# Attention tiles on TensorE: the transposes of tile n put in front of the score products of tile n+2

## The chip, the cores and the metric

The kernel runs on one core of a Trainium2 chip. The metric is the time of one execution in device microseconds (us); lower is better. The profile is one execution taken by the hardware profiler, and its times are in us from the first instruction of that execution.

## What is computed

A bucketed attention over 16 heads (2 batches of 8) with 768 positions and a head width of 64, and two dense layers behind it. Cut to what matters here:

```python
q_bits = (einsum(q, proj) > 0); k_bits = (einsum(k, proj) > 0)   # 6 bits: the bucket
mask   = q_bucket[:, None] == k_bucket[None, :]
scores = where(mask, q @ k.T / 8, -1e9)
attn   = exp(scores - max(scores)) / (sum + 1e-9)
x      = attn @ v                                                # 16 heads
x      = spatial gated MLP(x);  out = x + channel MLP(layernorm(x))
```

Products are made in three parts from high and low halves of the operands (names with h and l), so that they keep more digits than one pass would.

## The kernel before

**Tiles.** A head has 768 queries, that is T = 6 tiles of 128; the 16 heads give 96 tiles, numbered here from 0 to 95. Two heads are a pair of TILES = 12 tiles. HC = 3 tiles make half a head. Everything of the attention is written as one software pipeline over tiles, and every engine has its own fixed order of instructions, a function `steps` that goes through the tiles; engines meet only at semaphores.

**What happens to a tile n.** TensorE makes its scores (`scores`, lines L495 and L496, four matmuls of 384 columns into two banks of PSUM; tiles n and n+2 share these banks). VectorE reads them once for the negated row maximum (`maximum`, L950). ScalarE makes the exponentials into `Pe` in SBUF (`exps`, L789, signalled by `exp_done`). TensorE transposes `Pe` in six pieces (`transposes`, L526) into two banks, PT_BANK and PT_BANK+1, three pieces to a bank. ScalarE copies each bank to `PTh` (L784), rounded; VectorE subtracts to get the rest, `PTl` (`pt_lo`, L971), one instruction a bank, each of which counts `pt_split` up and so sets the bank free for the next tile's transposes. TensorE multiplies both with V (`times_v`, L538 and L540, four matmuls in most steps, for the half head before).

**The order of each engine in step n.**

- TensorE: scores of tile n+2, transposes of tile n, in some steps hash products (L505, steps with n % 6 of 1 and 2) or the turn of an output (L549, n % 3 = 0), then `times_v`.
- VectorE: maximum of tile n+2, in some steps the denominator (L977, n % 3 = 2) and the sum of the bucket bits (L963, n % 6 = 3), then `pt_lo` of tile n, and behind it the inverse (L982) and the one-hot codes of the next head (L933 at n % 6 = 1, L941 at n % 6 = 2).
- ScalarE: exponentials of tile n+1, in some steps a copy of an output (L795), `PTh` of tile n, in some steps the scaling of an output (L803).
- GpSimd splits q, k, v and the weights of the later layers; the sync engine's queue loads them.

The waits at the heart of it are these:

```python
# TensorE, transposes of tile g (n = its number in the pair)
pe.wait_ge(exp_done, g + 1)
for j in range(2):
    pe.wait_ge(pt_split, START + 2 * g + j - 1)   # VectorE is done with bank j of tile g-1
# VectorE, steps
maximum(g0 + n + 2, (n + 2) % TILES)              # waits for scores_ready of tile n+2
...
pt_lo(g0 + n, n)                                  # waits for pt_hi (PTh) of tile n
```

Before step 0 TensorE makes the scores of tiles 0 and 1; the last two steps (94 and 95) make no scores.

Of the kernel before, what the change touches and what calls it, by code (L numbers as in the profile page):

```python
# [24 lines left out]
def bucket_attention_mlp_kernel(nc, bucket_rows, qkT, qqT, kkT, v, proj, w_in, w_spT, b_sp, w_out, g_ln, w_ch, consts, out):  # L25
# [20 lines left out]
    with ctx:  # L46
        def sem(name):
            return ctx.enter_context(nc.semaphore(name))
# [152 lines left out]
        exp_done = sem("exp_done")  # L201
# [277 lines left out]
        def _(pe):  # L479
# [6 lines left out]
            def scores(n, hh):  # L486

                s, t = n // T, n % T
                if t == 0:
                    pe.wait_ge(head_split, 7 * hh + 5)  # L490
                    pe.wait_ge(coded, 2 * (hh + 1))
                tok = slice(t * P, (t + 1) * P)
                for c in range(2):
                    dst = bank[:, 2 * (n % 2) + c, 0:C]
                    nc.tensor.matmul(dst, Qs[s][:, tok], KH[s][:, c * C:(c + 1) * C], start=True, stop=False)  # L495
                    last = nc.tensor.matmul(dst, Q2[s][:, tok], KL[s][:, c * C:(c + 1) * C], start=False, stop=True)  # L496
                last.then_inc(scores_ready, 1)

            def hash_planes(hh, tiles):


                if tiles[0] == 0:
                    pe.wait_ge(qk_in, 16 * (hh + 1))
                for t in tiles:
                    last = nc.tensor.matmul(bank[:, MISC, 2 * t * NB:2 * (t + 1) * NB],  # L505
                                            qk_raw[:, bass.ds(t, P, step=T)], planes[:, :], start=True, stop=True)
                if tiles[-1] == T - 1:
                    last.then_inc(hash_mm, 1)

            def spread_buckets(hh, s):  # L510

                pe.wait_ge(buckets, hh + 1)
                for a, to in ((1, misc16), (0, o16)):
                    for t in range(T):
                        last = nc.tensor.transpose(to[:, t * P:(t + 1) * P],
                                                   cols[:, s, a, t:t + 1].to_broadcast([P, P]), ident16[:, :])
                    last.then_inc(kb_mm, 1)

            def transposes(g, n):

                pe.wait_ge(exp_done, g + 1)
                for j in range(2):
                    pe.wait_ge(pt_split, START + 2 * g + j - 1)
                    for r in range(HC):
                        k = HC * j + r
                        last = nc.tensor.transpose(bank[:, PT_BANK + j, r * P:(r + 1) * P],  # L526
                                                   Pe[n % 2][:, k * P:(k + 1) * P], ident)
                    last.then_inc(pt_ready, 1)

            def times_v(g0, hh0, c, tiles):  # L530

                s, m = (c // 2) % 2, c % 2
                if tiles[0] == 0:
                    if m == 0:
                        pe.wait_ge(head_split, 7 * (hh0 + c // 2 + 1))
                    pe.wait_ge(pt_split, START + 2 * (g0 + HC * (c + 1)))
                for k in tiles:
                    nc.tensor.matmul(bank[:, O_BANK, 0:C], Vs[s][:, k, :], PTh[m][:, k, :],  # L538
                                     start=(k == 0), stop=False)
                    last = nc.tensor.matmul(bank[:, O_BANK, 0:C], Vs[s][:, k, :], PTl[m][:, k, :],  # L540
                                            start=False, stop=(k == T - 1))
                if tiles[-1] == T - 1:
                    last.then_inc(av_done, 1)

            def turn(cc):

                pe.wait_ge(o_copied, cc + 1)
                for r in range(HC):
                    last = nc.tensor.transpose(bank[:, MISC, r * P:(r + 1) * P], OTs[:, r * P:(r + 1) * P], ident)  # L549
                last.then_inc(o_turned, 1)  # L550

            def steps(pair, which, hashed, last=False, first=False):

                g0, cc0, hh0 = TILES * pair, 4 * pair, 2 * pair
                for n in which:
                    if n + 2 < TILES or not last:
                        pe.wait_ge(exp_done, g0 + n + 1)
                        scores((n + 2) % TILES, hh0 + (n + 2) // T)  # L560
                    transposes(g0 + n, n)
                    if first:
                        if n == 1:
                            spread_buckets(1, 1)
                        if n == 3:
                            pe.wait_ge(kb_copied, 4)
                            hash_planes(2, range(T))
                    elif n % T in (1, 2) and hashed:
                        if n % T == 1:
                            pe.wait_ge(o_scaled, START + cc0 + n // HC - 1)  # L570
                        half = n % T - 1
                        hash_planes(hh0 + n // T + 2, range(HC * half, HC * (half + 1)))
                    if n % HC == 0 and n >= 2 * HC:
                        if n % T == HC and hashed:
                            pe.wait_ge(bits_weighted, hh0 + n // T + 3)
                        else:
                            pe.wait_ge(o_scaled, START + cc0 + n // HC - 2)
                        turn(cc0 + n // HC - 2)
                    if last and n >= 3 * HC:
                        if n < TILES - 1:  # L580
                            times_v(g0, hh0, 2, range(HC * (n % HC), HC * (n % HC) + HC))
                    elif n >= HC:
                        times_v(g0, hh0, n // HC - 1, range(2 * (n % HC), 2 * (n % HC) + 2))
# [181 lines left out]
            for n in range(2):  # L765
                scores(n, 0)
            steps(0, range(1), False, first=True)
            pe.wait_ge(kb_copied, 2)
            hash_planes(1, range(T))
            steps(0, range(1, 4), False, first=True)  # L770
            with pe.Fori(0, NP - 2) as pair:
                steps(pair, range(4, TILES + 4), True)
# [446 lines left out]
```

## Time and profile before

| | before |
|---|---|
| time, median of 3 runs | 716.25 us (716.23 to 717.16) |
| time of the profiled execution | 717.95 us |
| its span, first to last instruction | 716.1 us |
| TensorE busy | 697.4 us, 97% of the span |
| VectorE busy | 363.0 us, 51% |
| ScalarE busy | 300.5 us, 42% |
| GpSimd busy | 307.1 us, 43% |
| mean granted TensorE clock | 0.995 |

The profiled execution took 1.85 us more than its span, which lie around the instructions. The attention fills roughly the first 282 us; the dense layers follow. A busy share over the whole span mixes these stages, so the stretch of the attention has to be read by itself. In the views PE is TensorE's matmuls, PEld its weight loads (which overlap the matmuls), DVE is VectorE, ACT is ScalarE and POOL is GpSimd. The end of a matmul in the records is modelled and lies behind the point where the next may begin: in a stream of them the distance from start to start tells the cost.

### The profile page before, as it was taken

What the parts mean: (1) busy time and instruction counts of PE and PEld (TensorE: products, weight loads), DVE (VectorE), ACT (ScalarE), POOL (GpSimd) and SP (SyncE); (2) the same over time, 40 slices, a digit from 0 to 9 for tenths busy, and PEclk for the clock granted to TensorE, in tenths of its full rate; (3) what the DMA queues carried; (4) which work ended last, traced back from release to release, by engine and by line L of the source; (5) the groups of instructions that cost most, each with busy time, mean ns of one, the idle gap of its engine ahead of it and who ended that gap; (6) DMA issues with size and microseconds to landing.
All of it is one profiled execution on the core that took longest, in us unless ns stands there. A gap on an engine that the chain in (4) does not pass through costs nothing.

```text
span 716.1 us, 12014 instructions
## 1 busy us (share of the span) xinstructions
PE 697.4 (97%) x3864; PEld 644.9 (90%) x3864; DVE 363.0 (51%) x812; ACT 300.5 (42%) x685; POOL 307.1 (43%) x312
## 2 busy tenths in 40 slices
PE   4999999999999999999999999999999999999998
PEld 3898899999999988899889989998899889999996
DVE  3589989989888896444551111114344551111113
ACT  2567788887878887331231111111241241111110
POOL 5847777777555631600024444441300014444441
PEclk9899999999999999999999999999999999999999
DMA  6333444544423200200001221113100002221112
GB/s 203 112 118 111 110 118 134 143 133 117 118 88 89 90 21 24 68 22 1 0 1 59 78 69 59 59 59 114 62 1 1 0 1 60 87 59 59 59 59 88
DMA packets 20651, 51.10 MB, mean 71 GB/s; under 512 B 4496, under 2 KB 6672, under 8 KB 20624
## 3 DMA queue, kind: packets, MB, share of 16 engines
q1 hardware_dynamic: 19280, 45.25, 21.0%
q0 software_dynamic: 1344, 5.51, 2.4%
q8 instruction: 15, 0.25, 0.1%
q14 instruction: 12, 0.10, 0.0%
HBM read 47.56 MB, written 3.19 MB: 71 GB/s over the span
## 4 chain that ended last, share of the span: by engine, by line
PE 91%; DVE 3%; issue 3%; ACT 1%; DMA 0%; DVEq 0%; SPq 0%
PE bank L700 13%; PE bank L726 12%; PE bank L526 8%; PE bank L482 7%; PE bank L484 7%; PE bank L483 7%; PE bank L705 6%; PE bank L730 6%; PE bank L505 5%; PE bank L495 4%; PE bank L538 4%; PE bank L496 4%; PE bank L540 4%; PE bank L549 2%; DVE PTl L971 1%
## 5 line engine op out<-in xcount | busy, mean ns | idle before, releaser
L1084 DVE SCALAR_TENSOR_TENSOR Hl<-bank,Hh 128x384 fp32r<-128x384 f32 x64 | 35.7, 558 | 208.6 <-ACT Hh L857 208.5
L358 POOL TENSOR_SCALAR W1h<-w_raw 128x512 fp32r<-128x512 f32 x32 | 19.9, 622 | 278.7 <-PE bank L705 218.9
L857 ACT ACTIVATE Hh<-bank 128x384 fp32r<-128x384 f32 x64 | 31.5, 492 | 216.1 <-PE bank L705 216.1
L950 DVE TENSOR_SCALAR_CACHE_REDUCE negated<-bank 128x768 bf16<-128x768 f32 x96 | 91.9, 957 | 30.1 <-PE bank L496 28.1
L784 ACT ACTIVATE PTh<-bank 128x384 fp32r<-128x384 f32 x192 | 84.9, 493 | 40.9 <-PE bank L526 40.6
L971 DVE TENSOR_TENSOR PTl<-bank,PTh 128x384 fp32r<-128x384 f32 x192 | 97.9, 550 | 2.2 <-ACT PTh L784 1.8
L789 ACT ACTIVATE Pe<-bank,neg_max 128x768 f32<-128x768 f32 x96 | 87.1, 908 | 13.8 <-DVE negated L950 13.3
L526 PE MATMUL bank<-cst,Pe 128*128 128x128 f32 x576 | 83.3, 280 | 3.8 <-DVE PTl L971 3.7
L700 PE MATMUL bank<-XNh,W1l 128*128 128x384 f32 x256 | 86.9, 339 | 0.0
L700 PE MATMUL bank<-XNh,W1h 128*128 128x384 f32 x256 | 86.7, 339 | 0.0
L526 PEld LDWEIGHTS bank<-cst,Pe 128*128 128x128 f32 x576 | 68.6, 143 | 12.9 <-DVE PTl L971 4.2
L495 PE MATMUL bank<-KH,Qs 128*128 128x384 f32 x192 | 67.8, 353 | 5.2 <-DVE KL L941 3.4
L538 PE MATMUL bank<-PTh,Vs 128*128 128x384 f32 x186 | 71.4, 384 | 0.0
L726 PE MATMUL bank<-W2l,Hh 128*128 128x512 f32 x180 | 70.9, 394 | 0.0
L726 PE MATMUL bank<-W2h,Hh 128*128 128x512 f32 x180 | 70.8, 393 | 0.0
L496 PE MATMUL bank<-KL,Q 128*128 128x384 f32 x192 | 66.8, 348 | 0.0
L540 PE MATMUL bank<-PTl,Vs 128*128 128x384 f32 x186 | 63.5, 341 | 0.0
L705 PE MATMUL bank<-XNl,W1h 128*128 128x384 f32 x256 | 54.7, 334 | 0.0
L700 PEld LDWEIGHTS bank<-XNh,W1h 128*128 128x128 f32 x256 | 48.1, 188 | 3.5 <-ACT XNh L851 0.7
L730 PE MATMUL bank<-W2h,Hl 128*128 128x512 f32 x180 | 51.2, 392 | 0.0
L700 PEld LDWEIGHTS bank<-XNh,W1l 128*128 128x128 f32 x256 | 48.0, 188 | 2.5
L505 PE MATMUL bank<-planes,qk_raw 128*128 128x12 f32 x192 | 44.6, 358 | 5.0 <-DMA planes<-proj 5.0
(120 smaller groups left out, 1418.6 us busy)
## 6 DMA issues: line engine op xcount, KB each, us to landing
w_raw<-w_ch SPq DMA_DIRECT2D x32, 512.0 KB, 3.5
qk_raw<-qkT SPq DMA_DIRECT2D x16, 384.0 KB, 4.4
q_raw<-qqT SPq DMA_DIRECT2D x16, 384.0 KB, 4.7
k_raw<-kkT SPq DMA_DIRECT2D x16, 384.0 KB, 5.2
v_raw<-v SPq DMA_DIRECT2D x16, 192.0 KB, 4.2
out<-X SPq DMA_DIRECT2D x12, 256.0 KB, 2.0
rows<-code_rows SPq DMA_DIRECT2D x14, 192.0 KB, 4.4
w_raw<-w_spT POOLq DMA_DIRECT2D x6, 384.0 KB, 3.3
```

The lines of the kernel that those rows point to most:

```text
L495: nc.tensor.matmul(dst, Qs[s][:, tok], KH[s][:, c * C:(c + 1) * C], start=True, stop=False)
L496: last = nc.tensor.matmul(dst, Q2[s][:, tok], KL[s][:, c * C:(c + 1) * C], start=False, stop=True)
L526: last = nc.tensor.transpose(bank[:, PT_BANK + j, r * P:(r + 1) * P], Pe[n % 2][:, k * P:(k + 1) * P], ident)
L538: nc.tensor.matmul(bank[:, O_BANK, 0:C], Vs[s][:, k, :], PTh[m][:, k, :], start=(k == 0), stop=False)
L540: last = nc.tensor.matmul(bank[:, O_BANK, 0:C], Vs[s][:, k, :], PTl[m][:, k, :], start=False, stop=(k == T - 1))
L700: nc.tensor.matmul(bank[:, h_bank, 0:C], w1[s][:, k * P:(k + 1) * P], XNh[:, k, c * C:(c + 1) * C], start=(k == j == 0), stop=False)
L705: last = nc.tensor.matmul(bank[:, h_bank, 0:C], W1h[s][:, k * P:(k + 1) * P], XNl[:, k, c * C:(c + 1) * C], start=False, stop=(k == KD - 1))
L726: nc.tensor.matmul(bank[:, t, :], Hh[s][:, t * P:(t + 1) * P], w2[s][:, :], start=first and k == 0, stop=False)
L730: last = nc.tensor.matmul(bank[:, t, :], Hl[s][:, t * P:(t + 1) * P], W2h[s][:, :], start=False, stop=False)
L789: nc.scalar.activation(Pe[n % 2][:, :].rearrange("p (c n) -> p c n", c=2), bank[:, 2 * (n % 2):2 * (n % 2) + 2, 0:C], ACT.Exp, bias=neg_ma ...
L950: nc.vector.tensor_scalar(halves(negated[:, :]), bank[:, 2 * (n % 2):2 * (n % 2) + 2, 0:C], -SCALE, 3.0e38, ALU.mult, ALU.min, accum_out=n ...
L971: nc.vector.tensor_tensor(PTl[m][part], bank[:, PT_BANK + j, 0:C].rearrange("p (k q) -> p k q", k=HC), f32(PTh[m][part]), ALU.subtract).th ...
```

## The change

Within a step the transposes of tile n are issued ahead of the score products of tile n+2. The wait for `exp_done` that stood in front of the scores goes, since `transposes` begins with the same wait. No instruction that computes is added or removed, and no other engine's order is touched.

```diff
                 for n in which:
+                    transposes(g0 + n, n)
                     if n + 2 < TILES or not last:
-                        pe.wait_ge(exp_done, g0 + n + 1)
                         scores((n + 2) % TILES, hh0 + (n + 2) // T)
-                    transposes(g0 + n, n)
                     if first:
```

## Rows read from the trace of the kernel before

**Rows 1.** The page's chain that ended last, share of the span by engine.

```profile
PE 91%; DVE 3%; issue 3%; ACT 1%; DMA 0%; DVEq 0%; SPq 0%
```

**Rows 2.** Busy time by stretch; the first line names the columns.

```profile
core 0: us, PE busy (x) PEld busy (x) DVE busy (x) ACT busy (x) POOL busy (x), PEclk, DMA share, GB/s
27.00:30.00 3.00, 1.54 (x10) 1.00 (x9) 2.45 (x5) 2.92 (x7) 1.06 (x2) 1.00 0.43 164
...
33.00:36.00 3.00, 3.00 (x11) 2.90 (x12) 0.61 (x3) 0.12 (x2) 2.92 (x2) 0.50 0.28 9
...
159.56:166.35 6.79, 6.79 (x42) 6.72 (x41) 6.25 (x14) 4.76 (x11) 4.26 (x5) 1.00 0.31 91
39.80:274.20 234.40, 231.27 (x1476) 220.84 (x1475) 211.24 (x496) 192.46 (x469) 151.14 (x149) 1.00 0.36 103
0.00:39.80 39.80, 28.41 (x134) 26.55 (x135) 18.42 (x37) 16.44 (x30) 26.04 (x28) 0.91 0.51 163
274.20:716.10 441.90, 437.74 (x2258) 397.54 (x2256) 133.30 (x281) 91.56 (x187) 129.96 (x135) 1.00 0.14 46
```

**Rows 3.** Waits, 39.8 to 274.2 us: total us, times, longest us.

```profile
ACT PTh L784 <- PE bank L526: 32.2, 47, 1.6
...
DVE negated L950 <- PE bank L496: 20.8, 44, 1.3
...
PE bank L526 <- DVE PTl L971: 3.0, 4, 0.8
```

**Rows 4.** Line L950, maxima of tiles 7 to 95: ns, first and last start.

```profile
L950 DVE TENSOR_SCALAR_CACHE_REDUCE negated<-bank x89: 947/958/960, 39.8 to 274.2; 128x768 bf16<-128x768 f32 x89
```

**Rows 5.** Timeline, steps 45 to 47: start, length, instruction, [idle before <-releaser].

```profile
150.85 0.96 DVE L950 TENSOR_SCALAR_CACHE_REDUCE negated<-bank 128x768 bf16<-128x768 f32 x1
...
151.99 1.01 DVE L971 TENSOR_TENSOR PTl<-bank,PTh 128x384 fp32r<-128x384 f32 x2
...
152.64 0.97 PE L526 MATMUL bank<-cst,Pe 128*128 128x128 f32 x6
...
153.06 0.31 PEld L526 LDWEIGHTS bank<-cst,Pe 128*128 128x128 f32 x3 [0.15 <-DVE PTl L971]
...
153.06 0.96 DVE L950 TENSOR_SCALAR_CACHE_REDUCE negated<-bank 128x768 bf16<-128x768 f32 x1
...
153.36 0.42 PE L538 MATMUL bank<-PTh,Vs 128*128 128x384 f32 x1
...
153.62 0.33 PE L540 MATMUL bank<-PTl,Vs 128*128 128x384 f32 x1
...
153.94 1.02 DVE L971 TENSOR_TENSOR PTl<-bank,PTh 128x384 fp32r<-128x384 f32 x2
...
154.15 0.34 PE L495 MATMUL bank<-KH,Qs 128*128 128x384 f32 x1
...
154.86 0.82 PE L526 MATMUL bank<-cst,Pe 128*128 128x128 f32 x6
...
155.27 0.96 DVE L950 TENSOR_SCALAR_CACHE_REDUCE negated<-bank 128x768 bf16<-128x768 f32 x1 [0.31 <-PE bank L496]
...
155.43 0.42 PE L538 MATMUL bank<-PTh,Vs 128*128 128x384 f32 x1
...
156.23 1.02 DVE L971 TENSOR_TENSOR PTl<-bank,PTh 128x384 fp32r<-128x384 f32 x2
```

**Rows 6.** Timeline, VectorE in step 49, with the longest one-hot code.

```profile
160.86 1.02 DVE L971 TENSOR_TENSOR PTl<-bank,PTh 128x384 fp32r<-128x384 f32 x2
...
161.91 1.65 DVE L933 TENSOR_SCALAR Q<-rows,own 64x768 fp32r<-64x768 bf16 x1
...
163.59 0.96 DVE L950 TENSOR_SCALAR_CACHE_REDUCE negated<-bank 128x768 bf16<-128x768 f32 x1
```

**Rows 7.** Timeline, step 4, where the clock is at half.

```profile
34.61 0.52 PE L495 MATMUL bank<-KH,Qs 128*128 128x384 f32 x1
...
36.36 0.96 DVE L950 TENSOR_SCALAR_CACHE_REDUCE negated<-bank 128x768 bf16<-128x768 f32 x1 [2.41 <-PE bank L496]
```

## The prediction

> **What bounds the kernel now.** I read the chain that ended last first: 91% of it is TensorE [rows 1]. Then the busy time by stretch, since one share over the span says nothing of the attention. From 39.80 to 274.20 us, the steady part of it, TensorE is busy 231.27 of 234.40 us, VectorE 211.24 and ScalarE 192.46 [rows 2]. So TensorE sets the pace, but VectorE has only 10% to spare: the reader should carry that into everything below. Third the waits of the same stretch: TensorE waits 3.0 us for VectorE's split of the banks, while ScalarE waits 32.2 us for transposes and VectorE 20.8 us for scores [rows 3]. The others wait for TensorE. Last the timeline of three steps, for the distances in time that a busy share doesn't show [rows 5]. The pace is read from the maxima: 89 of them, of tiles 7 to 95, start from 39.8 to 274.2 us [rows 4], so 88 steps in 234.4 us, 2.66 us a step. Plain steps are shorter, 152.64 to 154.86 from transposes to transposes, 2.22 us, and hash steps longer.
>
> **The change part by part.** Removed: one wait for the exponentials a step, which cost nothing beside the same wait in the transposes. Moved: in 94 steps (0 to 93) four score matmuls go behind six transposes. The work of TensorE is the same, so its own sum doesn't move. No DMA is issued in what is moved, and neither the sync queue nor GpSimd's is passed. What changes is what waits for what.
>
> VectorE's order is maximum of tile n+2, then the split of tile n. Its order stays. Before, the chain from the split of tile n-1 led to the transposes of n, through ScalarE to the split of n, and the maximum stood outside this chain, as its scores had been issued ahead of the transposes. After, the scores of n+2 stand behind the transposes of n, and these wait until VectorE has split tile n-1 in the same bank. VectorE can't start the split of n before it has done the maximum of n+2. That closes a ring in every step: split of n-1, transposes of n, scores of n+2, maximum of n+2, split of n. Two tiles of lead in the scores don't help, because the ring doesn't go through the lead but through the order of VectorE. Round it once, each link from a row:
>
> 1. From the end of the split's second bank to the next TensorE instruction behind the second three transposes. The pair of splits at 151.99 ends at 153.01 (the row says 1.01, so 153.00); the weight load released by it starts at 153.06 and the matmul behind the transposes at 153.36 [rows 5]: 0.35 us.
> 2. From the first score matmul to the maximum: 154.15 to 155.27, where the maximum had waited for it: 1.12 us. Behind transposes the first matmul holds the next back: 153.36 to 153.62 is 0.26, against about 0.18 for each of four from 154.15 to 154.86. That adds 0.08: 1.20 us.
> 3. From the maximum's start to the split's: 153.06 to 153.94, 0.88 us.
> 4. The two splits, 1.02 us.
>
> The sum is 3.45 us a step, against 2.22 for the plain step. TensorE's other work goes beside it: after the scores (0.8 us) it has 2.3 us until the split ends, and `times_v` takes 0.8 of it. A hash step adds 3.4 less 2.2, that is 1.2 us, also there; TensorE's own work in it, 159.56 to 166.35 for two such steps [rows 2], is 3.4 us a step, just under the ring. So in hash steps nothing is added to 3.45, and they lose almost nothing; if the two don't interleave, I bound that at 0.1 us for each of 26 hash steps, 3 us. ScalarE's exponentials and copies are 192.46/88 = 2.2 us a step [rows 2] and begin as soon as the maximum before and the first transposes are done; they lie beside the ring.
>
> What stands on VectorE between maximum and split lengthens the ring: the sum of the bits, 150.85 to 151.99 is 1.14 instead of 0.88, 0.26 in 13 steps, 3.4 us; the denominator, 155.27 to 156.23 is 0.96, 0.08 in 29 steps, 2.3 us [rows 5]. What stands behind the split is covered while TensorE does links 1 and 2, 1.55 us. The long one-hot code needs 161.88 to 163.59, 1.71 us [rows 6], so 0.16 in 14 steps, 2.2 us; the short one is covered.
>
> The stretch of rows 4 becomes 88 x 3.45 + 7.9 = 311.5 us, which is 77.1 more than 234.4. Ahead of it, TensorE is busy 28.41 of 39.80 us [rows 2] and the steps already wait for the start of data; the first six moves can cost nothing or, at the 1.2 us of a plain step, 7. I take 1, as these steps are mostly longer than 3.45. The dense layers behind it, 441.90 us [rows 2], only begin later. At the end, tiles 94 and 95 have no scores; their transposes come a little earlier behind the last maximum, which I take at -0.5 (bounds -1 and +1.2). Together +77.6: the profiled execution's 717.95 becomes 795.5, and the median, 1.7 lower at 716.25, becomes 793.9. I predict 794.
>
> Bounds of the step. From below: if only the first bank's split bound, the ring would be 0.05 + 0.57 (all six transposes, 154.86 to 155.43) + 1.20 + 0.88 + 0.51 = 3.21 us [rows 5], 88 x 0.24 = 21 less: 773. From above: if the links each lose a little to one another and hash steps add theirs, 3.60 us, 13 more, and the start's 6: 813. I stay at 3.45, as both of its waits are seen in rows at this very place.
>
> **The rivals.** *The clock falls.* In a plain step TensorE would work 2.2 of 3.45 us. In this trace it was busy 1.54 of 3.00 us from 27 us on, and from 33 to 36 us the granted clock is 0.50, the 1.2 GHz level [rows 2]. At that level link 2 is 34.61 to 36.36, 1.75 us [rows 7], with 0.15 for the first matmul, and link 1 about 0.6: 0.6 + 1.9 + 0.88 + 1.02 = 4.4 us a step. All 88 steps at it would be 84 us more, 878; half of them 836. Against it: hash steps hold the same score, transpose and value matmuls in 3.4 us plus very short ones, and there the clock is 1.00 [rows 2]; a 3.45 us step has nearly the same matmuls in nearly the same time. I give it 0.13. The Trainium skill, "TensorE: Matmul & The Clock Gate", under "A second HAM failure mode: psum-queue depth-cycling", warns that frequent short idle times between groups of matmuls make the clock swing between its levels; by that rule this rival would be the likelier one, and the row at 33 us agrees that idle can bring the fall, while the hash steps' row speaks against it at this share of work.
>
> *No change.* TensorE's order is only permuted and its 231.27 us stay. If scores had slack enough, 716. It would need the ring to be shorter than TensorE's own step, 2.2 to 3.4 us; the ring's VectorE part alone is 1.9 us. It decides only if VectorE could run the split ahead of the maximum, and the rows show it in the program's order every time [rows 5]. 0.03.
>
> *Faster.* The transposes come 0.71 us sooner, and ScalarE's 32.2 us of waits for them go [rows 3]; if the split came sooner by as much, TensorE's 3.0 us would vanish too, 713. The point from which it decides is that the maximum of n+2 must be able to end before `PTh` of n is ready. The maximum began 0.41 us behind the start of the transposes (154.86 to 155.27); after the change it can't begin before 1.7 us behind it (0.57 + 1.20). 0.02.
>
> *A cheaper ring*, 3.0 us or less a step by links that overlap in a way that these rows don't show: 88 x 0.45 less, 754 or below. 0.05.
>
> **How the numbers follow.** The forecast, 773 to 813, has 0.77; the clock 0.13; a cheaper ring 0.05; no change 0.03; faster 0.02. The range 776 to 828 takes in most of the forecast's, 0.75, and the clock's case where it falls in a minority of steps, 0.05. A difference of 0.2% is 1.4 us, about what a measurement of this kernel can tell from none. Faster 0.02, the same 0.03, slower 0.95.
>
> **What would show it.** Right: the maxima of tiles 7 to 95 spread over about 312 us, plain steps and hash steps both near 3.45 us; VectorE idle between split and maximum, its wait for scores up from 20.8 us to over 80; TensorE waiting for the split in nearly every step, where it waited 4 times [rows 3], with a total of some 70 to 80 us; busy time of VectorE unchanged; the stretch behind the attention as long as before. A granted clock under 1.00 there would show the clock rival. The prediction is wrong if plain steps stay near 2.2 us (the ring isn't closed), if they are well under 3.2 (a link is shorter), or if ScalarE's copy is what the split waits for.

## The result, and the profile after

The changed kernel takes 795.24 us (median of 4 runs, 794.63 to 797.84) against 716.7 us for the kernel before on the same chip (4 runs): a ratio of 1.110, 95% interval 1.107 to 1.113. The median rose by 78.5 us; the prediction was 794. The profiled execution took 795.49 us with a span of 793.7 us, 77.6 us more than the span before, which is the sum that was predicted.

In the changed kernel most lines of the profile lie one lower than before: the maximum is L949, the split L970, the exponentials L788, the copies to `PTh` L783. The page first, busy time and the chain that ended last by engine:

```profile
PE 715.4 (90%) x3864; PEld 634.8 (80%) x3864; DVE 352.5 (44%) x812; ACT 308.8 (39%) x685; POOL 307.6 (39%) x312
...
PE 82%; DVE 8%; issue 7%; DVEq 1%; ACT 1%; DMA 0%; SPq 0%
```

TensorE's share of the chain fell from 91% [rows 1] to 82%, and VectorE's rose from 3% to 8%: part of the chain now runs through VectorE. Busy time by stretch, with the columns of [rows 2], for the maxima of tiles 7 to 95 and for what lies behind them:

```profile
40.97:351.84 310.87, 250.30 (x1478) 212.47 (x1477) 200.04 (x497) 200.98 (x469) 153.10 (x149) 1.00 0.27 77
351.84:793.70 441.86, 437.10 (x2252) 396.82 (x2250) 133.25 (x280) 90.47 (x184) 129.70 (x135) 1.00 0.14 46
```

The steady stretch grew from 234.4 to 310.87 us, while the dense layers take what they took, 441.86 against 441.90 us. TensorE, which had 3 us of idle time in this stretch, now has 60.6. The granted clock is 1.00. The line of the maxima, as in [rows 4], and the waits of the stretch, as in [rows 3]:

```profile
L949 DVE TENSOR_SCALAR_CACHE_REDUCE negated<-bank x89: 957/958/959, 41.0 to 351.8; 128x768 bf16<-128x768 f32 x89
```

```profile
DVE negated L949 <- PE bank L496: 110.6, 89, 1.6
...
PE bank L526 <- DVE PTl L970: 60.6, 62, 1.3
...
ACT PTh L783 <- PE bank L526: 4.9, 15, 0.4
```

The two engines wait for each other. VectorE's wait for scores went from 20.8 us in 44 steps to 110.6 us in all 89; TensorE's wait for the split from 3.0 us in 4 places to 60.6 us in 62. ScalarE's wait for the transposes nearly vanished, 32.2 to 4.9 us: the gain that the move does bring, and worth nothing here. The ring itself can be read from one step of the timeline, with its columns as in [rows 5]:

```profile
207.85 0.96 DVE L949 TENSOR_SCALAR_CACHE_REDUCE negated<-bank 128x768 bf16<-128x768 f32 x1 [1.57 <-PE bank L496]
...
208.73 1.02 DVE L970 TENSOR_TENSOR PTl<-bank,PTh 128x384 fp32r<-128x384 f32 x2
...
209.34 0.31 PEld L526 LDWEIGHTS bank<-cst,Pe 128*128 128x128 f32 x3 [1.36 <-DVE PTl L970]
209.34 1.01 PE L526 MATMUL bank<-cst,Pe 128*128 128x128 f32 x6 [1.04 <-DVE PTl L970]
...
209.80 0.31 PEld L526 LDWEIGHTS bank<-cst,Pe 128*128 128x128 f32 x3 [0.15 <-DVE PTl L970]
...
210.11 0.42 PE L495 MATMUL bank<-KH,Qs 128*128 128x384 f32 x1
...
211.31 0.96 DVE L949 TENSOR_SCALAR_CACHE_REDUCE negated<-bank 128x768 bf16<-128x768 f32 x1 [1.56 <-PE bank L496]
```

Follow it round: maximum at 207.85, splits at 208.73 (0.88), which end at 209.75 (1.02); the second three weight loads at 209.80 and the scores at 210.11 (0.36); the next maximum at 211.31 (1.20). That is 3.46 us, the four links of the prediction at 0.88, 1.02, 0.35 and 1.20.

### The profile page after: what moved, and what is told of

It is laid out like the page before. It is cut to its first block, busy times and chain, and to the rows that moved or that the text cites. A ratio compares the mean times of both kernels' runs of the same rounds, so it can differ in the third digit from the quotient of the medians.

```text
span 793.7 us, 12014 instructions
## 1 busy us (share of the span) xinstructions
PE 715.4 (90%) x3864; PEld 634.8 (80%) x3864; DVE 352.5 (44%) x812; ACT 308.8 (39%) x685; POOL 307.6 (39%) x312
## 4 chain that ended last, share of the span: by engine, by line
PE 82%; DVE 8%; issue 7%; DVEq 1%; ACT 1%; DMA 0%; SPq 0%
PE bank L526 12%; PE bank L699 11%; PE bank L725 11%; PE bank L482 7%; PE bank L484 7%; PE bank L483 7%; PE bank L704 6%; PE bank L729 5%; PE bank L505 5%; PE bank L496 4%; PE bank L495 4%; DVE PTl L970 4%; DVE negated L949 3%; PE bank L538 2%; PE bank L540 1%
## 5 line engine op out<-in xcount | busy, mean ns | idle before, releaser
L526 PE MATMUL bank<-cst,Pe 128*128 128x128 f32 x576 | 95.5, 292 | 65.4 <-DVE PTl L970 64.6
L949 DVE TENSOR_SCALAR_CACHE_REDUCE negated<-bank 128x768 bf16<-128x768 f32 x96 | 92.0, 958 | 121.7 <-PE bank L496 121.7
L526 PEld LDWEIGHTS bank<-cst,Pe 128*128 128x128 f32 x576 | 61.2, 143 | 104.7 <-DVE PTl L970 72.0
L788 ACT ACTIVATE Pe<-bank,neg_max 128x768 f32<-128x768 f32 x96 | 86.7, 903 | 96.6 <-DVE negated L949 96.6
L970 DVE TENSOR_TENSOR PTl<-bank,PTh 128x384 fp32r<-128x384 f32 x192 | 97.6, 550 | 1.9 <-ACT PTh L783 1.8
L783 ACT ACTIVATE PTh<-bank 128x384 fp32r<-128x384 f32 x192 | 89.2, 493 | 12.6 <-PE bank L526 8.1
L495 PE MATMUL bank<-KH,Qs 128*128 128x384 f32 x192 | 74.9, 390 | 3.4 <-DVE KL L940 3.4
L538 PE MATMUL bank<-PTh,Vs 128*128 128x384 f32 x186 | 68.0, 366 | 0.0
L368 POOL TENSOR_TENSOR X<-On 128x192 f32<-128x192 f32 x32 | 19.0, 593 | 102.8 <-ACT On L802 102.8
```

The lines of the kernel that those rows point to most:

```text
L783: nc.scalar.activation(dst, src, ACT.Copy).then_inc(done, 1)
L788: nc.scalar.activation(Pe[n % 2][:, :].rearrange("p (c n) -> p c n", c=2), bank[:, 2 * (n % 2):2 * (n % 2) + 2, 0:C], ACT.Exp, bias=neg_ma ...
L949: nc.vector.tensor_scalar(halves(negated[:, :]), bank[:, 2 * (n % 2):2 * (n % 2) + 2, 0:C], -SCALE, 3.0e38, ALU.mult, ALU.min, accum_out=n ...
L970: nc.vector.tensor_tensor(PTl[m][part], bank[:, PT_BANK + j, 0:C].rearrange("p (k q) -> p k q", k=HC), f32(PTh[m][part]), ALU.subtract).th ...
```

## Experiments

**The same work at two places of VectorE's order.** A memset of 128x512 that nobody reads was added to every step of the changed kernel, once between maximum and split and once behind the split:

```diff
...                                    # the tile idle_tile and the semaphore extra_done are set up
+            def extra(g):
+                dve.wait_ge(extra_done, START + g)
+                passed(dve)
+                nc.vector.memset(idle_tile[:, :], 0.0).then_inc(extra_done, 1)
...
+                    extra(g0 + n)          # extra_ahead
                     pt_lo(g0 + n, n)
+                    extra(g0 + n)          # extra_behind
```

> The changed kernel with one more VectorE instruction in every step (a memset of a tile of 128x512 that nobody reads), put between the maximum of tile n+2 and the split of tile n. Ring theory: this place lies on the ring, so every one of some 90 steps gets longer by the whole length d of the instruction as the trace shows it: pitch 3.46 + d, time 795 + 94 d; for d between 0.2 and 0.5 us that is 814 to 842 us. Rival (VectorE has idle time to give, 122 us of it ahead of its maxima, so what is added there is absorbed): 795 us.

> The changed kernel with the same additional VectorE instruction, but behind the split of tile n. Ring theory: here it lies beside TensorE's transposes and scores, for which VectorE waits about 1.56 us in a plain step; only where the one-hot code stands as well can a little stick out. Time 795 to 798 us, though VectorE does exactly the work of the run before it. Rival (VectorE's amount of work sets the pace): as long as that run, 814 to 842 us.

The memset is the same in both runs; this is the line of the first:

```profile
L970 DVE MEMSET idle_tile<- x96: 485/485/485, 20.9 to 403.6; 128x512 f32 x96
```

Ahead of the split the kernel takes 842.85 us, 47.6 more than the changed kernel; 96 x 0.485 is 46.6. The plain step went from 3.46 to 3.94 us. Behind the split it takes 798.27 us, 3.0 more (its two runs, 796.59 and 799.96 us, lie 3.4 us apart; the profiled one is the slower), with the plain step still at 3.46; only one step of each head, where the inverse, the bits and the short one-hot code stand behind the split as well, grew, from 3.66 to about 3.96. Even that isn't the memset alone. In the changed kernel VectorE still has 0.70 us of idle time in this step, more than 0.485; but pushed back by the memset, the short code meets one of GpSimd's subtractions and takes 1.07 to 1.12 us instead of 0.62. Together that is 0.3 us too much for the gap. So the same 46.6 us of VectorE's work cost all or nearly nothing by their place. VectorE's amount of work isn't the bound, and the split lies on the ring.

**Half of the transposes ahead of the scores.**

```diff
...                                    # transposes takes the banks that it fills as an argument
-                    transposes(g0 + n, n)
+                    transposes(g0 + n, n, (0,))
                     if n + 2 < TILES or not last:
                         scores((n + 2) % TILES, hh0 + (n + 2) // T)
+                    transposes(g0 + n, n, (1,))
```

> In every step TensorE makes the first three transposes of tile n, then the scores of tile n+2, then the last three transposes. Ring theory: the second of the two splits leaves the ring; it is then 0.05 + 0.30 + 1.20 + 0.88 + 0.51 = 2.94 us. Plain steps 2.95 us, hash steps 3.4 us (TensorE's own work), per head 2 x 3.4 + 4 x 2.95 + 0.4 = 19.0 us against 21.3: 761 us, between 755 and 768. Rival (what costs is the loss of the scores' lead over the transposes as such, so half of the transposes ahead cost half): 756 us with plain and hash steps both near 3.0. Rival (any transposes ahead of the scores cost it all): 795 us.

It takes 761.0 us, ratio 1.063 (1.060 to 1.066). Its timeline, in a step with the denominator ahead of the split:

```profile
192.26 1.02 DVE L972 TENSOR_TENSOR PTl<-bank,PTh 128x384 fp32r<-128x384 f32 x2
...
192.86 0.31 PEld L527 LDWEIGHTS bank<-cst,Pe 128*128 128x128 f32 x3 [1.11 <-DVE PTl L972]
...
193.17 0.42 PE L495 MATMUL bank<-KH,Qs 128*128 128x384 f32 x1
...
194.37 0.96 DVE L951 TENSOR_SCALAR_CACHE_REDUCE negated<-bank 128x768 bf16<-128x768 f32 x1 [1.01 <-PE bank L496]
...
195.25 1.01 DVE L972 TENSOR_TENSOR PTl<-bank,PTh 128x384 fp32r<-128x384 f32 x2
```

The transposes start at 192.86, in the middle of the pair of splits, which ends at 193.28: now only the first split is in the ring, and the step from split to split is 2.99 us. Plain steps are 2.99 to 3.00 us and hash steps 3.38 to 3.40 (3.46 and 3.32 in three early heads, with the same sum), where TensorE's own work binds. Somewhat under half of the loss, 34 of 78.5 us, came back: one split of 0.51 us left the ring, and the plain step fell by 0.47. The rival with 3.0 us in hash steps too is out.

**VectorE's order turned as well,** once in the changed kernel and once in the kernel before:

```diff
+                    pt_lo(g0 + n, n)
                     if n + 2 < TILES or not last:
                         maximum(g0 + n + 2, (n + 2) % TILES)
                     ...
-                    pt_lo(g0 + n, n)
```

> The changed kernel, and VectorE's order turned too: split of tile n, then maximum of tile n+2. Ring theory, traced further: the first ring is open, but another closes, since ScalarE makes the exponentials of n+1 ahead of its copies of n: maximum of n+1 to exponentials 1.01, to the copies 0.82, the two copies 0.89, to the end of the second split 0.55: 3.27 us, with 0.49 more in every third step for the copy of an output; hash steps 3.4. Per head 20.9 us against 21.3: 789 us, between 775 and 795. Rival (VectorE's order is all there is, and with it turned TensorE sets the pace again): 716 to 725 us.

> The kernel before (scores, then transposes), with only VectorE's order turned: split of tile n, then maximum of tile n+2. If the second ring (maximum of n+1, exponentials of n+1, copies of n, splits of n, maximum of n+2; 3.27 us) is what holds the kernel with both orders turned, this one holds just as long, as TensorE isn't in that ring: 780 to 795 us. If TensorE's order were what costs, this is as fast as before, 716 to 725 us.

The first takes 788.04 us, ratio 1.101 (1.099 to 1.103), the second 791.41 us, ratio 1.105 (1.102 to 1.108). Both have steps of 3.33, 3.34 and 3.71 us, whichever order TensorE has. The profiled execution of the second has a few longer ones as well, up to 4.11 us; there the granted clock fell, as told under the clock below. The timeline of the first shows the ring that took over:

```profile
190.00 0.95 DVE L949 TENSOR_SCALAR_CACHE_REDUCE negated<-bank 128x768 bf16<-128x768 f32 x1
...
190.99 0.90 ACT L788 ACTIVATE Pe<-bank,neg_max 128x768 f32<-128x768 f32 x1 [1.58 <-DVE negated L949]
...
191.88 0.86 ACT L783 ACTIVATE PTh<-bank 128x384 fp32r<-128x384 f32 x2
...
192.39 1.02 DVE L970 TENSOR_TENSOR PTl<-bank,PTh 128x384 fp32r<-128x384 f32 x2 [0.47 <-ACT PTh L783]
...
193.33 0.95 DVE L949 TENSOR_SCALAR_CACHE_REDUCE negated<-bank 128x768 bf16<-128x768 f32 x1
```

Maximum, exponentials, copies, splits, and the next maximum 3.33 us later, with TensorE in none of the waits. The simple reading, that the split should go first once the transposes do, is wrong: ScalarE makes the exponentials ahead of its copies, so VectorE's new order closes a ring with that. And the kernel before was fast because its maximum stood first, not in spite of it.

**All three orders turned.** The same edit, and in ScalarE's steps `exps` of tile n+1 behind the copies of tile n:

```diff
-                    if n + 1 < TILES or not last:
-                        exps(g0 + n + 1, (n + 1) % TILES)
...                                                  # copies to PTh of tile n
+                    if n + 1 < TILES or not last:
+                        exps(g0 + n + 1, (n + 1) % TILES)
```

> All three engines turned alike: TensorE transposes of n then scores of n+2, VectorE split of n then maximum of n+2, ScalarE copies of n then exponentials of n+1. Both rings are open; what is left is exponentials of n, transposes of n, copies of n, exponentials of n+1: 1.05 + 0.50 + 0.89 = 2.44 us, more in every third step for ScalarE's copy and scaling (3.3 to 3.8), hash steps 3.4. Per head 18.7 us: 758 us, between 740 and 770. Rival (a third ring as long as the others): 785 to 800 us. Rival (the orders only have to agree): 716 to 722 us.

It takes 723.24 us, ratio 1.010 (1.008 to 1.012), far below the 740 to 770 that I expected and next to the range of the rival by which the orders only have to agree, 716 to 722. The plain step was forecast well, 2.46 us against 2.44:

```profile
152.84 0.91 ACT L788 ACTIVATE Pe<-bank,neg_max 128x768 f32<-128x768 f32 x1
...
153.97 0.87 PE L526 MATMUL bank<-cst,Pe 128*128 128x128 f32 x6 [0.17 <-ACT Pe L788]
...
154.54 0.88 ACT L783 ACTIVATE PTh<-bank 128x384 fp32r<-128x384 f32 x2 [0.71 <-PE bank L526]
...
155.30 0.91 ACT L788 ACTIVATE Pe<-bank,neg_max 128x768 f32<-128x768 f32 x1
```

What I missed is that every third step isn't longer: ScalarE's copy and scaling of an output fall into its wait of 0.71 us for the transposes and into the hash steps. Most heads take 16.3 to 16.6 us (three early ones 17.2 to 17.4), not 18.7, so 758 was too high by 35 us. Most of the loss thus came from the transposes' new place against the orders of the two other engines: with these turned too, 7 us of it are left. No run shows a gain from the move.

**The move in some steps only.**

```diff
-                    transposes(g0 + n, n)
+                    early = n % T in (1, 2)          # hash_steps_only; not in (1, 2): other_steps_only
+                    if early:
+                        transposes(g0 + n, n)
                     if n + 2 < TILES or not last:
+                        if not early:
+                            pe.wait_ge(exp_done, g0 + n + 1)
                         scores((n + 2) % TILES, hh0 + (n + 2) // T)
+                    if not early:
+                        transposes(g0 + n, n)
```

> Transposes ahead of the scores in the hash steps only (n % 6 of 1 and 2), the old order in the others. Ring theory: the ring of 3.46 us lies beside 3.4 us of TensorE's own work, so almost nothing is lost: 717 to 725 us. Rival (each moved step costs alike): 32 of 94 steps, 743 us.

> Transposes ahead of the scores in all steps but the hash steps. Ring theory: nearly the whole loss lies here, 770 to 787 us. Rival (each moved step costs alike): 62 of 94 steps, 768 us.

In the hash steps alone the time is 723.4 us, ratio 1.010 (1.009 to 1.012), far from the 743 us of an equal price for each step. In all the others it is 777.1 us, ratio 1.084 (1.082 to 1.087); there the two theories had said 770 to 787 and 768, so this run alone would tell them apart only weakly. With the move in hash steps only these are 3.46 us long. In the profiled execution the last maximum starts 4.3 us later than before, and three parts of that can be read. The ten heads of tiles 24 to 83 take 16.4 us each, 0.4 more than before: 0.16 in the hash steps, the rest in the steps behind them. The last two heads have the move but no hash products beside it, and there these steps take 3.4 us; the two heads became 3.6 us longer together, as the ring says. Against that, three early heads became 3.5 us shorter together, with one-hot codes of 1.50 to 1.58 us instead of 2.37; the next part is about these. The two losses, 7.2 and 60.9 us, add to 68, not 78.5. With the move in the other steps only, one step of each head, where the order changes, is as short as 1.81 us: there the ring isn't closed. That this is all of the difference wasn't tested.

**GpSimd's order.** The changed kernel's VectorE was busy 10.5 us less than before, which no step of the prediction had. The one-hot codes had become short. A row of the kernel before and two of the changed kernel:

```profile
160.97 1.84 POOL L361 TENSOR_TENSOR WspL<-w_raw,WspH 128x768 fp32r<-128x768 f32 x1
```

```profile
196.28 1.82 POOL L361 TENSOR_TENSOR WspL<-w_raw,WspH 128x768 fp32r<-128x768 f32 x1
...
198.94 0.99 DVE L932 TENSOR_SCALAR Q<-rows,own 64x768 fp32r<-64x768 bf16 x1
```

Before, the code starts at 161.91 [rows 6], within GpSimd's subtraction, which ends at 162.81, and takes 1.65 us; after, it starts at 198.94, 0.84 us behind the subtraction's end, and takes 0.99. Two runs move GpSimd's work instead of TensorE's:

```diff
+                split_v(hh, s)
                 if 1 <= hh <= KD + T:
                     split_piece(hh - 1)
-                split_v(hh, s)
```

> The kernel before, with GpSimd's order changed: the split of a piece of the later layers' weights stands behind the split of v instead of ahead of it. In the trace of before, the one-hot code takes 2.37 us in three heads and about 1.7 in six, where it lies beside GpSimd's subtraction of such a piece, and 0.95 in five where it doesn't. Theory (the two shut each other out): moved away, most codes take 0.95 to 1.3 us; in the first three heads VectorE's delay reaches TensorE, 17.1 us a head against 15.9, so up to 1.1 us a head come back there and 0.1 to 0.2 in the six others: 712 to 714 us. Rival (the long codes are long for another reason, such as where they read, or cost nothing): 716 us, lengths as before.

> The changed kernel with the same turn in GpSimd's order. There VectorE waits 1.56 us behind its splits and all the codes are already short (0.94 to 1.00 us), so the ring sets the time as before: 794 to 796 us. If what GpSimd does mattered to the ring, it would move by more than 2 us.

In the kernel before this gives 712.5 us, ratio 0.995 (0.994 to 0.997), a gain of 0.5% and the one version that beats both kernels. Of the nine long codes one became 0.95 us, five 1.08 to 1.37 and three 1.75 to 1.90, since they now lie beside another of GpSimd's subtractions; a tenth grew from 0.95 to 1.36. The median fell from 1.65 to 1.11 us:

```profile
L933 DVE TENSOR_SCALAR Q<-rows,own x16: 620/1106/1898, 11.1 to 250.7; 64x768 fp32r<-64x768 bf16 x16
```

In the profiled execution the three heads that had held the 2.37 us codes became 4.8 us shorter together, more than the 1.1 us each that I had expected at most, and the heads behind them stayed within 0.3 us of what they were. In the changed kernel the same edit gives 796.88 us (2 runs, 795.83 to 797.93), against 794.63 to 797.84 for the four runs without it: 0.9 above the range that I had expected, but less than the 2 us that would speak for an effect. Its steps are the same, 3.46 and 3.66 and 3.72 us, since the ring doesn't pass through GpSimd.

## Why the prediction was right, point by point

- *What bounds it.* Right: TensorE bound before, and the busy shares hid the ring. VectorE was busy 90% of the stretch before and 64% after (200.04 of 310.87 us), and the kernel was slower; what counts is where its work stands, as the two memset runs show.
- *The ring's links.* 3.46 us measured against 3.45. The assumption that carries it, that VectorE never runs the split ahead of the maximum, held in every step read.
- *Hash steps.* Right in size: 3.46 us, 0.08 over TensorE's own 3.38; the second one of each head takes 3.66, for the denominator. The run with the move in these steps alone says that about 0.25 us a head can follow in the steps behind, where the order is the old one.
- *What stands between maximum and split.* The sum of the bits cost 0.26 (a step of 3.72), as said. The denominator cost 0.08 in one of its two places and 0.20 in the hash step, where it started 0.12 us later; 1.7 us more than in the sum.
- *The long one-hot code.* Wrong: I took 1.71 us from a row in which GpSimd stood in its way, and put 2.2 us on it. It took 0.94 to 1.00 us in the changed kernel and was covered.
- *The sum.* The stretch came to 310.87 us, forecast 311.5. From the steps read, the difference is +0.9 for the links, +1.7 for the denominator, -2.2 for the long code and -0.9 for the last 18 steps, which are 0.05 us shorter each (see the end of this document). The start gave 1.17, forecast 1, but not for the reason given: between the maxima of tiles 1 and 7 only three of six steps had been longer than 3.45 us, and the six changed by -0.6 to +1.2 us. Behind the last maximum nothing changed, forecast -0.5. That the total of 77.6 us is met to a tenth is luck in the small terms; the 88 x 3.45 is not.
- *The clock.* This rival did not come: granted clock 1.00 over the stretch, with TensorE busy 250.30 of 310.87 us. The warning of the Trainium skill ("TensorE: Matmul & The Clock Gate", "A second HAM failure mode: psum-queue depth-cycling") about short idle times between groups of matmuls was not borne out by this row, at about 1 us of idle time a plain step. It isn't out for every order of this kernel, though. In the profiled execution of `before_split_first` the granted clock did fall to half in the attention and came back: it reads 0.57 from 168 to 170 us, 0.50 from 188 to 190 and 0.50 from 334 to 336. Ahead of these, TensorE had been busy 2.88 of 5.00 us (160 to 165), 0.68 of 2.00 (184 to 186) and 1.12 of 2.00 (330 to 332). The longer steps of that run lie in these places; how much of their length is the clock's wasn't separated.
- *What would show it.* VectorE's wait for scores was to be over 80 us and was 110.6. TensorE's was to be 70 to 80, in nearly every step, and is 60.6 as idle time, in 62 places for 88 steps. VectorE's busy time was to stay and fell by 10.5 us. ScalarE's copy was not what the split waited for.
- *No change and faster.* Ruled out as stated: TensorE's order being only permuted doesn't help when another engine's fixed order closes a ring with it.

## What to carry to other kernels

When you move an instruction on one engine, list the fixed orders of all the engines that it exchanges buffers with, and look for a closed path through them; add its links from rows and compare the sum with the step of the engine that binds. A lead of two tiles in the data is no lead if a third engine serves both tiles in a fixed order. Idle time of an engine can absorb work only at the places that lie beside the path: here 0.485 us cost 47.6 us in all at one place and 3.0 us at another.

## What the runs showed of the hardware

A VectorE instruction that reads and writes SBUF only, the long one-hot code, took 0.94 to 1.00 us in the changed kernel with none of GpSimd's subtractions beside it, and 1.64 to 2.38 us in the kernel before where it met one. The maximum, which reads PSUM, stayed at 0.93 to 0.96 us in every run. The Trainium skill, "SBUF — State Buffer", "SBUF: two separate sides", says that the two engines share a pair of ports, and that the instruction which starts first holds it for its whole length, when the VectorE instruction is in a two-port mode or has two inputs in SBUF. No row shows the mode of the code, but the hold itself can be read from the rows. In the kernel before and in `before_piece_later` nine codes each met a subtraction. They started between 0.3 and 1.7 us ahead of its end and always ended 0.72 to 0.78 us behind it. Had the two shared the ports, a longer time side by side would have left less to do afterwards. By an estimate from these rows, only some 0.2 of the code's 0.95 us could go beside the subtraction. It goes the other way round too: GpSimd's rounding of V, 0.50 us elsewhere, took 0.93 us where it started 0.07 us behind the short code at 101.92 us of the kernel before.

Steps written out behind the loops are shorter than the same steps inside: 3.40 to 3.41 against 3.46 us from tile 78 on in the changed kernel, and 3.88 against 3.94 in the run with the memset ahead of the split. In the changed kernel the scores lead to the maximum there in 1.13 to 1.15 instead of 1.20 us. In the run with halved transposes no such difference is seen (3.00 and 2.99). What causes it was not tried and stays open.
